# The first chunk's token-major rows are loaded ahead of the second quarter of w_out2 and w3T

## What is computed

```python
B, H, S, D = 4, 8, 768, 48
for t in range(S):
    cur = einsum('bhd,bhe->bhde', u[None] * k_t, v_t)
    y[:, :, t] = einsum('bhd,bhde->bhe', r_t, state + cur)
    state = w_t[:, :, :, None] * state + einsum('bhd,bhe->bhde', k_t, v_t)
x = y as (B*S, H*D) = (3072, 384)
h = x @ w_in                                  # d_ff 2048
x = (h * clip(h + 3, 0, 6) / 6) @ w_out
out = ((x @ w1) * (x @ w2)) @ w3 @ w_out2     # d_ff 1024
```

## Time and profile before

| | before |
|---|---|
| median of 3 runs | 921.59 us (918.28 to 923.42) |
| profiled execution | 919.46 us |
| its span, first to last instruction | 917.7 us |
| PE busy | 893.5 us (97%) |
| DVE busy | 556.3 us (61%) |
| ACT busy | 316.7 us (35%) |
| POOL busy | 266.0 us (29%) |
| mean granted TensorE clock | 0.994 |

### The profile page before, as it was taken

The page is one execution under the profiler, slowest core; times in us unless marked ns, Lnnn a source line. Parts: engine busy times, 40 slices in busy tenths (PEclk is TensorE's granted clock), DMA queues, the critical chain, the costliest instruction groups (busy, mean ns, idle before and its releaser), DMA issues.

```text
span 917.7 us, 22942 instructions
## 1 busy us (share of the span) xinstructions
PE 893.5 (97%) x9988; PEld 805.8 (88%) x9988; DVE 556.3 (61%) x746; ACT 316.7 (35%) x532; POOL 266.0 (29%) x209
## 2 busy tenths in 40 slices
PE   8997989999999999999999999999999999999998
PEld 4555989999999999999999999998888888888887
DVE  5999987878787887878788853552222232222221
ACT  0324443343433344343434343542132222222212
POOL 0565646363636363636363600000000000000000
PEclk9999999999999999999999999999999999999999
DMA  9996524444344434343435101521020202000000
GB/s 301 338 288 227 146 68 135 108 136 127 123 118 131 120 115 123 114 123 115 122 115 137 36 20 39 191 82 52 1 69 1 69 1 70 0 35 1 8 28 34
DMA packets 62483, 93.29 MB, mean 102 GB/s; under 512 B 7928, under 2 KB 48463, under 8 KB 62383
## 3 DMA queue, kind: packets, MB, share of 16 engines
q1 hardware_dynamic: 59390, 88.16, 31.7%
q10 hardware_dynamic: 2992, 3.67, 1.4%
HBM read 76.07 MB, written 11.01 MB: 95 GB/s over the span
## 4 chain that ended last, share of the span: by engine, by line
PE 82%; DVE 9%; DMA 3%; issue 3%; POOL 1%; SPq 1%; ACT 1%; ACTq 0%; DVEq 0%
PE ps_acc L1101 11%; PE ps_acc L1103 10%; PE ps_acc L1102 10%; PE ps_h L1103 10%; PE ps_h L1102 10%; PE ps_h L1101 10%; PE ps_lv L1138 4%; PE ps_lv L1102 4%; PE ps_lv L1103 4%; PE ps_lv L1101 4%; DMA tok_a<-in_k 3%; DVE k_sb L810 2%; DVE A_own L922 2%; PE ps_acc L1176 1%; POOL tok_a L544 1%
## 5 line engine op out<-in xcount | busy, mean ns | idle before, releaser
L544 POOL TENSOR_TENSOR tok_a<-tok_a 128x384 f32<-128x384 f32 x126 | 164.1, 1330 | 185.8 <-DMA tok_a<-in_k 185.8
L587 ACT ACTIVATE g_hi<-gated 128x512 fp32r<-128x512 f32 x144 | 91.0, 632 | 241.7 <-PE ps_acc L1103 126.7
L1101 PE MATMUL ps_acc<-g_hi,w_out_hi 128*128 128x256 f32 x576 | 171.7, 298 | 0.0
L1102 PE MATMUL ps_acc<-g_hi,w_out_lo 128*128 128x256 f32 x576 | 163.3, 284 | 0.0
L1103 PE MATMUL ps_acc<-g_lo,w_out_hi 128*128 128x256 f32 x576 | 163.2, 283 | 0.0
L1101 PE MATMUL ps_h<-x_hi,w_in_hi 128*128 128x256 f32 x576 | 162.2, 282 | 0.9 <-DVE gated L1000 0.9
L1102 PE MATMUL ps_h<-x_hi,w_in_lo 128*128 128x256 f32 x576 | 161.9, 281 | 0.0
L1103 PE MATMUL ps_h<-x_lo,w_in_hi 128*128 128x256 f32 x576 | 161.8, 281 | 0.0
L1083 DVE TENSOR_TENSOR gated<-gated,ps_lv 128x512 f32<-128x512 f32 x48 | 33.1, 689 | 186.3 <-PE ps_lv L1103 186.3
L1101 PEld LDWEIGHTS ps_acc<-g_hi,w_out_hi 128*128 128x128 f32 x576 | 109.9, 191 | 5.2 <-issue 1.7
L1103 PEld LDWEIGHTS ps_acc<-g_lo,w_out_hi 128*128 128x128 f32 x576 | 110.2, 191 | 0.0
(11 more groups left out here) (99 smaller groups left out, 1620.0 us busy)
## 6 DMA issues: line engine op xcount, KB each, us to landing
tok_a<-in_r SPq DMA_DIRECT2D x21, 768.0 KB, 4.0
tok_a<-in_w SPq DMA_DIRECT2D x21, 384.0 KB, 4.8
v_sb<-in_v SPq DMA_DIRECT2D x12, 384.0 KB, 4.2
x_scratch<-x_out SPq DMA_DIRECT2D x12, 384.0 KB, 4.3
x_in<-x_scratch SPq DMA_DIRECT2D x6, 768.0 KB, 6.0
tok_a<-in_k SPq DMA_DIRECT2D x22, 192.0 KB, 5.0
out<-x_out SPq DMA_DIRECT2D x5, 768.0 KB, 4.0
x_sb<-y_sb SPq DMA_DIRECT2D x138, 24.0 KB, 2.2
```

The lines of the kernel that those rows point to most:

```text
L544: return nc.gpsimd.tensor_tensor(dst, x, y, ALU.mult)
L587: return nc.scalar.activation(dst, src, ACT.Copy, **scale)
L1101: nc.tensor.matmul(psum, hi, moving_hi, start=start, stop=False)
L1102: nc.tensor.matmul(psum, lo, moving_hi, start=False, stop=False)
```

## The change

`load_tok(0)` is issued one place earlier, between the two quarters. Nothing else is touched: the same 375 DMAs of SP with the same sizes, and no wait added or taken away.

```diff
             load_w(0)
             load_k(0)
             load_r(0)
             load_quarter(0)
+            load_tok(0)
             load_quarter(1)
-            load_tok(0)
             load_tok(1)
             load_w_over(1)
             load_k(1)
```

## The result

| | before | changed |
|---|---|---|
| median of 13 runs each | 920.02 us (915.96 to 923.81) | 925.22 us (921.28 to 930.05) |
| profiled execution | 919.46 us | 922.97 us |
| its span | 917.7 us | 921.1 us |
| PE busy | 893.5 us | 892.6 us |
| DVE busy | 556.3 us | 549.8 us |

The changed kernel is **slower: ratio 1.0057, 95% interval 1.0037 to 1.0078**. The difference of the medians is 5.2 us; the forecast was +4.8, and its time, 925.3.

The account below looks back on a forecast made before the run. PE, busy 893.5 of 917.7 us, was taken as the bound, so only the loop's start could move. 3.28 - 0.81 + 2.0 + 1.5 - 1.2 = +4.8 us gave 925.3 us, range 920.5 to 930.0.

Parts of the forecast that it names:

- The exchange itself: Head loads: in a saturated queue, exchanging two entries speeds neither up; the five transfers together end where they ended, 24.66.
- DVE's gain, spent waiting: Chunk 0's products on DVE start 2.9 us earlier, but all of it is spent waiting for PE before scale(0, 5).
- +3.28 for the quarter: PE, form_w34(0, 1): the second quarter lands at 24.66 in place of 21.38, 3.28 us later.
- -0.81 for the slack: PE, quarter to new states: the 0.81 us it waited before, for the turn at 34.86, absorbs part of the lateness.
- +2.0 for the clock: PE behind its 5.5 us idle: the granted clock falls to 0.50, costing 2.0 us (0 to 2.9).
- +1.5 for POOL beside DVE: DVE's scale(1, 1) moves wholly into POOL's work on chunk 2 and slows by 1.5 us (0 to 1.7).
- -1.2 for what comes back: Up to chunk 4: SP's wait and POOL meeting DVE less return 1.2 us (between 0 and 3.2).
- The rivals that the queue or DVE's head start decides: Queue swallows lateness by chunk 4's load: 0 to +1.5 us, chance 0.12; DVE's earlier sums make it faster: -2.9, chance 0.06.

Follow-up runs that it names:

- e4_order: The changed kernel with PE's list rearranged so that less stands between the second quarter and the turn (attention(0, 3) ahead of form_w34(0, 1)); ratio to before 0.9972.
- e3_later: The changed kernel with the second quarter loaded one place later still, behind both load_tok(0) and load_tok(1); ratio to before 1.0100.
- e8_pool_wait_before: The kernel before, with POOL's products for chunk 2 held back until scale(1, 1) is done; ratio to before 0.9977.
- e5_fill6: The changed kernel with six dummy matmul pairs, results unread, ahead of form_w34(0, 1) to keep PE busy while it waits for the quarter; ratio to before 1.0029.
- e2_pool_wait: The changed kernel with POOL's products for chunk 2 held back until scale(1, 1) is done; ratio to before 1.0032.
- e10_fill_before: The kernel before, with two dummies (1.8 us of unread matmuls) in PE's wait for the second quarter; ratio to before 0.9995.
- e6_order_before: The kernel before, old load order, with PE's and ACT's lists rearranged to put less behind the quarter, form_w34(1, 0) ahead of attention(0, 4); ratio to before 0.9975.

## Why the prediction was right

**The exchange itself.** Right. The five transfers ended nearly where they had: 24.66 before, 25.5 now. Of these 0.8 some 0.7 were there before the quarter mattered: `scale(0, 2)` already began at 13.46, against 12.79, behind loads that the change doesn't touch. Such a shift of the whole head is scatter between executions: in the twelve traces that start lies between 12.79 and 13.61, and at 12.90 to 13.33 in the three other kernels with the old order of loads.

**DVE's gain, spent waiting.** Right, but not the whole: chunk 0's products began 2.3 earlier (2.9 forecast) and ended at 25.75, and DVE then waited 5.02 for step 3, where the forecast's times (25.1 to 28.1) leave 3.0. e4_order shows the reason for the wait. The forecast left its own term for the clock out at this place: `scale(0, 5)` came at 30.77 and not at 28.1, and `sum_bands(0)` 3.6 late (32.88 against 29.26) and not "at most 0.2". With it POOL's chunk 2 did not stay at 42.4 but began at 44.11, since the load was issued 3.6 later and landed 1.7 later. This cost nothing in the sum only because `scale(1, 1)`, from 46.65 on, still fell wholly into POOL's 44.11 to 52.05.

**+3.28 for the quarter, -0.81 for the slack.** Right in kind, and the largest part. The profile gives 4.24 for the landing as PE saw it, with the scatter just named, and the wait of 0.81 for the turn is gone. e3_later shows that PE has no slack left for more lateness. With the other two terms cured, the total is 2.3 us over the kernel before and 4.4 over e8_pool_wait_before, where +3.28 - 0.81 forecast +2.5: a cost is shown, its size isn't fixed by them.

**+2.0 for the clock.** Right in kind, too large. The granted clock fell while PE stood idle for 5.81 us, and `form_w34(0, 1)` took 4.35 in place of 2.82: 1.5. e5_fill6 puts it at 1.2 on the path. The price differed from run to run: in the changed kernel and in e2_pool_wait, whose programs are the same up to there, the eight matmuls took 4.35 and 4.83 behind waits of 5.81 and 5.83. That agrees with the Trainium skill ("TensorE: Matmul & The Clock Gate", Part 1), by which the gate's watch runs free of the kernel's start. In e3_later and e4_order, with other waits ahead (10.54 and 3.35), they took 5.25 and 4.87.

**+1.5 for POOL beside DVE.** Right on the path up to sum_bands(1): from 46.65 to 50.15 `scale(1, 1)` took 3.50, against 2.35 before, so 1.15. What it was worth in the total stays open: with POOL's wait in both kernels the exchange costs 0.55%, and 0.57% without. The exclusive port pair of the Trainium skill ("SBUF — State Buffer", Who interferes with whom) agrees with the switch between 0.69 and 1.48 when POOL is held back. Not every row beside POOL is slow, though: at 37.70, with POOL at work from 34.73 to 39.23, `k_sb`'s product in `scale(0, 6)` took 0.68.

**-1.2 for what comes back.** Too much: 0.7 came back. sum_bands(1) was 6.2 late (6.0 forecast), chunk 4's issue 4.8, its landing 4.6: so 1.6 came back by then, 1.0 of it in `start(1)` (1.34 in place of 2.35). But POOL's products for chunk 4, which by the forecast would meet DVE less, took 12.40 in place of 11.56, so 0.84 of it was lost again, and the turn was 5.4 late. The same products took 12.57 in e10_fill_before, whose time is that of before, so this loss may be scatter.

**The total.** Read from the two profiles, the terms are 4.24 - 0.81 + 1.5 + 1.15 - 0.7 = +5.4, with the 0.7 of scatter in the first; the forecast's sum was +4.8, and the medians give +5.2. The errors of the terms partly cancel. That the time itself came within 0.1 us of 925.3 is luck: it was reached from a base of 920.5, a guess between the profiled 919.46 and the 921.59 of three runs, while the median of the 13 is 920.02. The two profiled spans differ by only 3.4, mainly since the trace of before has a further half-clock stretch behind the turn (at 126.2, for 3.4 us of full work, so 1.7 us lost) that the other lacks; from the turn to the end they took 827.8 and 825.8. The medians of 13 runs, 5.2 apart, are the better measure. The rivals that the queue or DVE's head start decides are out, by the lateness that passed through in e3_later and by DVE's wait.

## What to carry to other kernels

Two loads that shared a saturated queue and were both waited for only traded lateness here. Before exchanging such loads, ask for each waiting engine what stands behind the wait in its list, and how far it runs before the other engine needs it. DVE's gain ended at its next wait for PE; PE's loss ran through nearly twenty microseconds of work. Changing the waiting engine's list (e4_order, e6_order_before) brought the kernel to about 0.25% under the one before with either order of the loads. A wait on PE that grows may also cost the clock behind it (1.2 to 1.5 us here), so its price can exceed its length. And an experiment that cures one term is worth a control on the kernel before: POOL's wait gained as much there, so its gain on the changed kernel says little of the change.

## What the runs showed of the hardware

- `copy_predicated` between SBUF tiles can be slowed beside POOL too: the two of `start(1)` took 1.34 us without it (changed kernel) and 2.38 with it (e2_pool_wait). But those of `start(0)` took 1.34 in the kernel before with POOL at work from 32.74 to 39.71; there POOL's four products took 6.97 us, against 4.93 for the same four of chunk 2. The reduction of 128x1536 took 1.73 to 1.75 in every case.
- The last of the five transfers landed at 24.66 and 25.5 in the two orders, with 0.7 of the difference in the head before them; a single profile's head can sit up to 0.8 us later than another's (12.79 to 13.61 for the start of `scale(0, 2)`).
- The clock can fall behind a short wait as well: in e6_order_before it was 0.55 behind 1.59 us of idle time and 64 small matmuls, in the kernel before 1.00 behind 2.24 us of idle time in the same region.
- A profile's reading of a point 90 us into the kernel scattered by 1.4 us between kernels of the same time (before and e10_fill_before).
